# Turning x at steps 10 to 12, q a tile ahead, and TensorE transposes for the second tile in a fused attention and two-stage MoE kernel

## What is computed

```python
# attention without a softmax; q, k, v: 8 x 8 heads x 576 x 64
kv  = einsum('bhsd,bhse->bhde', k, v)
out = einsum('bhsd,bhde->bhse', q, kv)
out = out / sqrt(mean(out * out, -1) + 1e-6) * g_norm
x   = out.transpose(0, 2, 1, 3).reshape(4608, 512)
# dense part, 512 -> 2048 -> 512
h = x @ w_in
x = (max(h, 0) + alpha * min(h, 0)) @ w_out
# routed part: one of 8 experts for each token, 512 -> 1024 -> 512
e = argmax(x @ w_gate)
out[t] = softmax(x @ w_gate)[t, e] * sigmoid(x @ w_output_gate)[t, e] * (relu(x[t] @ w1[e]) @ w2[e])
```

## Time and profile before

| | us |
|---|---|
| median of three runs | 1504.78 |
| all three | 1504.66, 1504.78, 1505.2 |
| the profiled execution, its own time | 1506.15 |
| its span, first to last instruction | 1504.3 |
| TensorE busy in the span | 1437.9 (96%) |
| VectorE busy | 766.7 (51%) |
| ScalarE busy | 481.5 (32%) |

### The profile page before, as it was taken

The page is one execution under the profiler, slowest core; times in us unless marked ns, Lnnn a source line. Parts: engine busy times, 40 slices in busy tenths (PEclk is TensorE's granted clock), DMA queues, the critical chain, the costliest instruction groups (busy, mean ns, idle before and its releaser), DMA issues.

```text
span 1504.3 us, 27183 instructions
## 1 busy us (share of the span) xinstructions
PE 1437.9 (96%) x8157; PEld 1241.1 (83%) x8158; DVE 766.7 (51%) x1901; ACT 481.5 (32%) x997; POOL 128.5 (9%) x143
## 2 busy tenths in 40 slices
PE   7698999999999999999999999999999999999997
PEld 6587888888888888888888888888888888888886
DVE  3476666566656566656566665654133114444411
ACT  3233232323222222222322221334233234444422
POOL 1000000000000000000000000121111111111111
PEclk8799999999999999999999999999999999999999
DMA  8545333122424331524230201534123114444410
GB/s 185 116 121 131 80 78 88 49 62 66 96 52 106 54 72 33 109 51 95 55 85 23 64 22 43 114 120 152 46 92 100 47 38 149 154 141 153 151 46 32
DMA packets 182098, 130.53 MB, mean 87 GB/s; under 512 B 98859, under 2 KB 153275, under 8 KB 182013
## 3 DMA queue, kind: packets, MB, share of 16 engines
q1 hardware_dynamic: 173196, 107.01, 28.2%
q0 software_dynamic: 7872, 21.09, 4.4%
q10 hardware_dynamic: 944, 1.33, 0.4%
HBM read 101.37 MB, written 29.30 MB: 87 GB/s over the span
## 4 chain that ended last, share of the span: by engine, by line
PE 79%; DVE 8%; ACT 5%; DMA 3%; issue 3%; SPq 1%; POOL 0%; ACTq 0%; DVEq 0%; POOLq 0%
PE psH L1423 21%; PE psAcc L1435 19%; PE psAcc L1550 15%; PE psH L1529 15%; PE psO L1375 2%; PE psO L1539 2%; ACT XG L757 2%; DVE AR L1081 2%; DVE XG L969 2%; ACT XG L698 2%; DVE AR L956 2%; PE psQ L1510 1%; PE psO L1351 1%; DVE AR L1084 1%; SPq L372 1%
## 5 line engine op out<-in xcount | busy, mean ns | idle before, releaser
L1423 PE MATMUL psH<-XG,W 128*128 128x384 f32 x2304 | 437.0, 338 | 21.3 <-DVE W L1054 12.6
L1435 PE MATMUL psAcc<-W,XG 128*128 128x512 f32 x1728 | 443.2, 401 | 10.7 <-DVE XG L1088 10.7
L1423 PEld LDWEIGHTS psH<-XG,W 128*128 128x128 f32 x2304 | 410.0, 189 | 41.5 <-issue 14.6
L1435 PEld LDWEIGHTS psAcc<-W,XG 128*128 128x128 f32 x1728 | 317.3, 189 | 83.1 <-DVE XG L1088 16.2
L757 ACT ACTIVATE XG<-AR 128x128 fp32r<-128x128 f32 (+1 forms) x384 | 132.6, 365 | 611.3 <-DVE AR L1084 585.8
L1529 PE MATMUL psH<-W,XG 128*128 (+1 forms) x996 | 250.3, 400 | 0.1
L1550 PE MATMUL psAcc<-W,XG 128*128 (+1 forms) x984 | 242.0, 395 | 0.1
L1081 DVE TENSOR_SCALAR AR<-psH,acol 128x384 f32<-128x384 f32 x192 | 118.0, 615 | 230.7 <-PE psH L1423 230.3
L1550 PEld LDWEIGHTS psAcc<-W,XG 128*128 128x128 f32 x984 | 181.6, 188 | 37.3 <-issue 0.5
L1529 PEld LDWEIGHTS psH<-W,XG 128*128 128x128 f32 x996 | 180.9, 188 | 36.8 <-issue 0.3
L1255 DVE TENSOR_TENSOR XG<-psO,XG 128x512 fp32r<-128x512 f32 x82 | 56.6, 691 | 216.3 <-ACT XG L811 216.3
(11 more groups left out here) (202 smaller groups left out, 805.8 us busy)
## 6 DMA issues: line engine op xcount, KB each, us to landing
AR<-in_moe_w_dram SPq DMA_DIRECT2D x68, 512.0 KB, 5.1
AR<-in_k_dram SPq DMA_DIRECT2D x16, 576.0 KB, 5.3
rows<-AR SPq DMA_DIRECT2D x36, 256.0 KB, 2.2
xr<-AR SPq DMA_DIRECT2D x33, 256.0 KB, 6.2
AR<-xr SPq DMA_DIRECT2D x132, 64.0 KB
AR<-rows SPq DMA_DIRECT2D x132, 64.0 KB, 2.1
AR<-in_v_dram SPq DMA_DIRECT2D x14, 576.0 KB, 7.2
AR<-in_q_dram SPq DMA_DIRECT2D x112, 48.0 KB, 2.2
```

The costliest lines, as they stand in the source:

```text
L1423: mm = pe.matmul(psH[f % 2][:, 0:TILE], w_in_v[:, wp, cc, f * P:(f + 1) * P], xT[:, b, xp, cc, :], start=(cc == 0 and (wp, xp) == PARTS[0] ...
L1435: mm = pe.matmul(psAcc[m][:, :], gT[:, f % 2, gp, m * P:(m + 1) * P], w_out_v[:, wp, f, :], start=(f == 0 and (gp, wp) == PARTS[0]), stop= ...
```

## The change

x of a later tile is turned in steps 10, 11 and 12 in place of 13, 14 and 15, and its low parts follow one step later, in steps 11, 12 and 13. The first third of q is turned at the end of step 15, a tile earlier than it was; the other two stay in steps 1 and 2. For tile 1 (a = 1) q comes as plain rows in four DMAs, in place of 32 with blocks, and TensorE transposes q in steps 4 to 6 and x in steps 13 to 15 of tile 0; the store and the fetch of x for that tile go away, and ScalarE copies the transposed q out of PSUM. Counts of the semaphores follow.

```diff
         def q_count(i, c):
-            return 1024 * i + (0, 512, 768)[c]
+            return 1024 * i + (0, 512, 768)[c] - 512
+        def x_at(before):
+            return 10 if before else 13
+        def o_rows(a, j):
+            return AR[:, KN + j * DM:KN + (j + 1) * DM] if a else o_sb[:, j, :]
+        def x_source(a, j):
+            return FIRST_X[j][:, :] if a == 0 else psY[:, :] if a == 1 else sq_sb
...
-            def load_q_rows():
+            def load_q_rows(c):
                 for j in range(TG):
-                    sp.dma_start(q_sb[:, j, :].rearrange("s (h d) -> s h d", h=H),
-                                 q[0, :, j * P:(j + 1) * P, :].rearrange("h s d -> s h d")).then_inc(q_in[j], 16)
+                    if c:
+                        sp.wait_ge(q_tr, j + 1)
+                    for bl, s0, p0, n in group_place(c, j):
+                        sp.dma_start(q_sb[p0:p0 + n, j, :].rearrange("s (h d) -> s h d", h=H),
+                                     q[bl, :, s0:s0 + n, :].rearrange("h s d -> s h d")).then_inc(q_in[j], 16)
...
             load_dense(4)
-            load_q(0, 1)
+            load_q_rows(1)
             for f in range(5, FC):
                 load_dense(f)
-                if f == FC - 2:
-                    turn_x(1)
...
-                else:
-                    fetch_x(1)
...
 # ScalarE
-            def qT_evacuate(j):
-                act.wait_ge(q_tr, j + 1)
-                nc.scalar.activation(first_qT[j], FIRST_QT[j][:, :].rearrange("p (c n) -> p c n", c=CH), ACT.Copy
+            def qT_evacuate(a, j):
+                act.wait_ge(q_tr, 3 * a + j + 1)
+                if a:
+                    act.wait_ge(o_mm, 3 * a + j)
+                nc.scalar.activation((qT if a else first_qT[j]),
+                                     (psQ if a else FIRST_QT[j])[:, :].rearrange("p (c n) -> p c n", c=CH), ACT.Copy
                                      ).then_inc(qT_first, 1)
...
+                    if not before and g == 0:
+                        qT_evacuate(1, 0)
                     if not before and g == 1:
                         kv_evacuate(3, 1, 1)
                     if ahead and g in (1, 2, 3):
                         o_evacuate(a, g - 1)
+                    if not before and g in (1, 2):
+                        qT_evacuate(1, g)
...
-                    if ahead and f in (13, 14, 15):
-                        x_evacuate(a, b, f - 13)
+                    if ahead and f - x_at(before) in (0, 1, 2):
+                        x_evacuate(a, b, f - x_at(before))
...
 # VectorE
-                    if ahead and g in (0, 1, 2):
-                        q_turn(*nxt(i, c), g)
+                    if before and ahead and f in (1, 2):
+                        q_turn(*nxt(i, c), f)
...
-                    if ahead and f in (13, 14, 15):
-                        x_turn(a, f - 13)
+                    if not before and f in (13, 14, 15):
                         x_low(a, (i + c + 1) % 2, f - 13)
+                    if before and ahead and f in (11, 12, 13):
+                        x_low(a, (i + c + 1) % 2, f - 11)
+                    if before and ahead and f in (10, 11, 12):
+                        x_turn(a, f - 10)
+                    if t + 2 < TILES and f == FC - 1:
+                        q_turn(*nxt(*nxt(i, c)), 0)
...
 # TensorE
-            def q_transpose(j):
-                pe.wait_ge(q_in[j], 16)
+            def q_transpose(a, j):
+                pe.wait_ge(q_in[j], 48 if a and j == 1 else 16 * (a + 1))
+                if a:
+                    pe.wait_ge(qT_first, 3 * a + j)
+                if a and j == 0:
+                    pe.wait_ge(kv_set, 3)
...
-            def x_transpose(j):
-                pe.wait_ge(xn_set, j + 1)
+            def x_transpose(a, j):
+                pe.wait_ge(xn_set, 3 * a + j + 1)
+                if a and j:
+                    pe.wait_ge(x_lo, 3 * a + j)
...
+                    if not before and g in (0, 1, 2):
+                        q_transpose(1, g)
                     if not before and g == 1:
                         k_times_v(3)
...
+                    if not before and s >= 13:
+                        x_transpose(1, s - 13)
```

More of the change, by code:

```diff
@@ L419, in _ @@
             load_rows(sp, k, 0, 1, k_first, kv_in_1)
-            load_q_rows()
+            load_q_rows(0)
             load_dense(0)
@@ L735, in _ @@
             act.wait_ge(lists_init, 16)
-            qT_evacuate(0)
-            qT_evacuate(1)
+            qT_evacuate(0, 0)
+            qT_evacuate(0, 1)
             o_evacuate(0, 0)
-            qT_evacuate(2)
+            qT_evacuate(0, 2)
             o_evacuate(0, 1)
@@ L948, in q_turn @@
                 dve.wait_ge(o_mm, 3 * a + j)
+                if a == 2 and j == 0:
+                    dve.wait_ge(qT_first, 2 * TG)
                 V.transpose(out=qT.rearrange("p c (t i) -> p c t i", i=32), in_=q_blocks[:, :, 4 * j:4 * j + 4, :]
@@ L952, in x_turn @@
             def x_turn(a, j):
-                dve.wait_ge(x_back[j], 64 * a)
+                dve.wait_ge(x_back[j], 64 * (a - 1))
                 dve.wait_ge(x_lo, 3 * a + j)
@@ L1354, in k_times_v @@
                 mm.then_inc(kv_mm, 1)
-            def q_transpose(j):
-                pe.wait_ge(q_in[j], 16)
+            def q_transpose(a, j):
[4 more added lines that the diff above has]
+                    pe.wait_ge(kv_set, 3)
+                bank = psQ if a else FIRST_QT[j]
                 for cc in range(CH):
-                    mm = pe.transpose(FIRST_QT[j][:, cc * P:(cc + 1) * P], q_sb[:, j, cc * P:(cc + 1) * P], ident[:, :])
+                    mm = pe.transpose(bank[:, cc * P:(cc + 1) * P], q_sb[:, j, cc * P:(cc + 1) * P], ident[:, :])
                 mm.then_inc(q_tr, 1)
@@ L1377, in q_times_kv @@
                 mm.then_inc(o_mm, 1)
-            def x_transpose(j):
-                pe.wait_ge(xn_set, j + 1)
+            def x_transpose(a, j):
+                pe.wait_ge(xn_set, 3 * a + j + 1)
+                if a and j:
+                    pe.wait_ge(x_lo, 3 * a + j)
+                bank = x_source(a, j)
                 for cc in range(CH):
-                    mm = pe.transpose(FIRST_X[j][:, cc * P:(cc + 1) * P], o_sb[:, j, cc * P:(cc + 1) * P], ident[:, :])
+                    mm = pe.transpose(bank[:, cc * P:(cc + 1) * P], o_rows(a, j)[:, cc * P:(cc + 1) * P], ident[:, :])
                 mm.then_inc(x_tr, 1)
@@ L1451, in _ @@
             k_times_v(1)
-            q_transpose(0)
-            q_transpose(1)
+            q_transpose(0, 0)
+            q_transpose(0, 1)
             q_times_kv(0, 0, 0, 2)
-            q_transpose(2)
+            q_transpose(0, 2)
             q_times_kv(0, 0, 1, 2)
@@ L1463, in _ @@
             for j in range(TG):
-                x_transpose(j)
+                x_transpose(0, j)
             k_times_v(2)
```

43 lines of the change are left out of this document (23 added, 20 removed).

## The result

| | before | after |
|---|---|---|
| median (four runs each, same chip) | 1504.72 us | 1460.06 us |
| all | 1504.21 to 1505.2 | 1458.74 to 1461.17 |
| the profiled execution, own time | 1506.15 | 1459.46 |
| its span | 1504.3 | 1457.6 |
| start of tile 0, of tile 1 | 31.34, 128.34 | 30.79, 114.75 |

A forecast was written before the change was run, and what follows sets the result against it. TensorE, busy nearly throughout, was held to be bounded by its own order and its waits in the dense part. 30.3 us (tiles 1 to 10) plus 11.7 (tile 0) made 42.0 less: 1462.5 us, range 1456 to 1472.

The forecast's parts named there:

- The boundary: From hidden(15) to the next tile's hidden(2): 16.51 us would become 13.48, 3.03 us won in each of ten tiles.
- slack of 0.17 us: Step 15: g would be there 4.03 us behind the start of hidden(15), output(15) being due at 4.20.
- Rival 2: Tile boundary stays tight: step 15's chain is late, output(15) still waits, 0.7 us less won each; 1470 us, chance 0.12.
- x's share and q's share: Of the 30.3 us in tiles 1 to 10, 18.8 from turning x earlier and 11.5 from q's first third.
- Piece 5: Tile 0's load_dense(5), behind q's loads: ScalarE starts at 51.0 instead of 60.94, a gain of 9.9 us (bounds 4.4 and 10.4).
- Rival 1: Tile 0 keeps its hole: q's row loads hold SP, load_dense(5) lands at 56.5, tile 0 gives about 5; 1469 us, chance 0.13.
- my two prices: Tile 0, q's row loads: at 232 GB/s load_dense(5) lands at 50.6; at the early row loads' issue times, 56.5.
- Step 5: Tile 0: 12.37 us would become 10.65, a gain of 1.7, with waits of about 1.3 and 2.0 us for ScalarE.
- The end of tile 0: Steps 13 to 15 would take 18.2 us in place of 20.2, a gain of 2.0, with 1.5 us of wait.
- the clock: Tile 0: waits of 1.3, 1.3 and 2.0 us within 10 us would lower TensorE's clock, charged once at 1.6 us.
- Rival 3: Slower: x not back at step 10 in six tiles; past 183 each us costs 6 us, 1509 at 191; chance 0.03.
- The sign that I had named: Step 10: the forecast would be wrong if VectorE waits there for x to come back.

The follow-up runs named there:

- x12: The changed kernel with x turned in steps 12 to 14 and its low parts in steps 13 to 15; 1463.98 us, ratio 0.9735 to the kernel before.
- after_again: The changed kernel itself, unchanged, run once more on the same chip beside later variants; 1460.08 us, ratio 0.9712 to the kernel before.
- q_behind5: The changed kernel with only load_dense(5) moved ahead of the row loads of q; 1460.29 us, ratio 0.9706 to the kernel before.
- x8: The changed kernel with x turned in steps 8 to 10 and its low parts in steps 9 to 11; 1479.03 us, ratio 0.9836 to the kernel before.
- order1: The changed kernel with tile 0's loads, copies and splits reordered, including load_dense(5) before q's rows and load_dense(4) before the last k and v load; 1458.23 us, ratio 0.9698.

## Why the prediction was right, point by point

- **The boundary** was forecast to go from 16.51 to 13.48 us; it is 13.41 to 13.44 in the nine from tile 1 to tile 10. The two at the ends have only one of the two waits each: from tile 10 to 11, with no q behind it, `hidden(15)` to `hidden(2)` went from 14.51 to 12.62, x's share alone, and q's tenth wait was in tile 1, behind the end of tile 0. Term 30.3, measured 31.3. That the slack of 0.17 us suffices is shown by step 15's chain, which begins at the 2.3 us that I had worked out, and x12 shows that it does even with work ahead of it. Rival 2 did not come.
- **x's share and q's share**: 18.8 and 11.5 forecast, 20.3 and 11.2 measured alone, each edit removing its own waits at the boundaries and no others.
- **Piece 5**: ScalarE was forecast to have it at 51.0 and had it at 51.45; `hidden(5)` at 53.65, and it came at 54.07, with 1.34 us of wait (1.3). `hidden(4)` to `hidden(5)` gained 9.8 (9.9). Rival 1 did not come. The four row loads did hold SP for 5.39 us, but none for more than 1.9; SP was free at 45.0, not at 51.4, and piece 5 reached ScalarE by the lower of my two prices.
- **Step 5**: forecast 10.65, measured 10.18; waits of 0.97 and 1.65 where I took 1.3 and 2.0. Step 6 grew by 0.44 (0.6).
- **The end of tile 0**: 17.72 (18.2), one wait of 1.65 (1.5). No run changes this part alone.
- **The one term that was wrong is the clock.** I charged 1.6 us for three waits within 10 us. In the stretch that holds them it did not fall, as this row of the kernel after shows (columns as in the earlier trace rows, the granted clock before the DMA share):

```profile
54.00:64.00 10.00, 7.31 (x80) 6.44 (x81) 5.48 (x13) 6.06 (x14) 0.00 (x0) 1.00 0.38 107
```

  The nine matmuls behind the wait for kv took 2.3 us in after_again and 3.74 in q_behind5. So such a charge can come, but need not, and I had no row that said so; that it did not come in either profile of the kernel after was luck as far as the prediction goes. The charge is more than the whole difference between the terms of tile 0, 11.7 forecast and 13.0 measured: steps 5, 6 and the end gave 4.3 us for the 3.1 of their terms, and 0.8 went into a longer wait before `hidden(4)` (1.83, before 1.03), which the change does not aim at. The 0.3 for the first pair behind tile 0 lies in tile 1.
- The rule of the Trainium skill (TensorE: Matmul & The Clock Gate, part 4, PE-mode transpose), by which transposes don't count as busy for the clock gate, would have kept steps 4 to 6 at half clock. The row above, with transposes in it, has 1.00, but it also holds k times v, `hidden` and `output`. A stretch of after_again ahead of tile 0 tells more. TensorE does nothing but transposes from 23.25 to 28.9 us, with the row's 24 and 12 more behind them, and the granted clock (same columns) goes from the lower of its two levels to the full one in the middle of them:

```profile
23.25 4.50 PE L1498 MATMUL psQ<-ident 128*128 128x128 f32 x24 [1.39 <-ACT acol L760]
```

```profile
23.50:26.90 3.40, 3.40 (x18) 3.40 (x17) 2.92 (x10) 0.74 (x2) 0.00 (x0) 0.50 1.09 196
26.90:31.50 4.60, 3.72 (x68) 3.41 (x66) 2.20 (x6) 2.84 (x8) 0.00 (x0) 1.00 0.42 92
```

  So here, for fp32 transposes of 128x128, the measurement goes against the rule.
- **Rival 3** had its mechanism right (x8), its price too high and its distance too large. I counted 2 us until TensorE feels it; it has 4.1. But I looked at the first third alone and gave it 2.6 us to spare, and in the kernel after VectorE did wait, in step 11 for the second third (0.60 us, tile 1, in one of two profiles). In tile 1 VectorE reaches the first turn 51.0 us behind the tile's start, where I had taken 52.8 from the kernel before: the tile has become shorter, its fetch of x has not become earlier (45.8 us behind the start, before 46.1). The sign that I had named came in a small way; the 4.1 us kept it from TensorE. A slip in the sum besides: at 6 us for each us past 183 a third landing at 191 gives 1510.5, not 1509.

## What to carry to other kernels

Ask of each wait which block stands between producer and consumer in the consumer's own order: work that is late by some us costs nothing where a whole block of TensorE lies in between, and all of it at the one place, as `output(15)` here, where that block is missing. Count the DMAs, and not only their bytes, that one queue issues ahead of a load that somebody waits for: with the same bytes 32 held SP for 18.75 us and four for 5.39. And when a stretch has several short waits, try to take them away together: one alone (q_behind5) gave nothing here, and one more load moved ahead (order1) pushed the wait to the data behind it.
